# Mixture-of-experts stage of one fused kernel: the first two work items take their rows by gathers alone, with a spare gather ahead

## The reference

```python
# 1: attention, 4 batches x 8 heads x 576 rows, head_dim 64
scores = scale * q @ k.T
scores = where(scores >= max(scores) - tau, scores, -1e9)
x = softmax(scores) @ v                       # then reshaped to 2304 tokens x 512
# 2: mixture of experts, one expert of 8 for each token
logits = x @ w_gate                           # 512 x 8
expert_idx = argmax(logits, axis=1)
gate_w = softmax(logits)[expert_idx]
for e in range(8):
    xe = x[expert_idx == e]
    out[expert_idx == e] = gate_w * (relu(xe @ w1[e]) @ w2[e])   # 512x1024, 1024x512
# 3: dense layer
h = x @ w_in                                  # 512 x 2048
out = (h - tanh(h)) @ w_out                   # 2048 x 512
```

## Time and profile before

| what | value |
|---|---|
| runs of the kernel before, median (lowest to highest) | 1090.57 us (1089.77 to 1091.09) |
| the profiled execution, its own time | 1086.2 us |
| its span, from the first to the last instruction | 1084.1 us |
| mean granted PE clock in it, of full speed | 0.991 |
| PE busy | 1042.3 us, 96% of the span |
| DVE, ACT, POOL busy | 673.7, 469.0, 785.4 us |
| DMA traffic | 110.01 MB, mean 101 GB/s |

### The profile page before, as it was taken

How to read it: one execution, slowest core, us unless ns; L and a number is a source line. 1 busy time by engine, 2 the same in 40 slices (tenths; PEclk the granted TensorE clock), 3 DMA queues, 4 the chain that set the end, 5 groups by cost and what they waited for, 6 DMA issues and landing times.

```text
span 1084.1 us, 18472 instructions
## 1 busy us (share of the span) xinstructions
PE 1042.3 (96%) x5928; PEld 869.4 (80%) x5929; DVE 673.7 (62%) x1396; ACT 469.0 (43%) x945; POOL 785.4 (72%) x794
## 2 busy tenths in 40 slices
PE   6999999999995989999999999999999999999997
PEld 5767767777774778888888888999999999999995
DVE  5777777777786132322234226997777777777775
ACT  5777777777763122222222224433343333333332
POOL 4788888666632867967899803888878778787885
PEclk9999999999998999999999999999999999999999
DMA  6464575554532555635564521010000100000000
GB/s 120 112 173 127 149 207 119 159 133 110 152 113 68 201 193 178 209 126 194 179 214 171 210 79 58 1 31 10 20 30 27 33 10 21 30 20 11 11 20 29
DMA packets 100487, 110.01 MB, mean 101 GB/s; under 512 B 64896, under 2 KB 64896, under 8 KB 99904
## 3 DMA queue, kind: packets, MB, share of 16 engines
q1 hardware_dynamic: 88160, 85.73, 27.3%
q10 hardware_dynamic: 9136, 13.15, 3.8%
q0 software_dynamic: 3120, 10.24, 2.5%
HBM read 68.01 MB, written 27.32 MB: 88 GB/s over the span
## 4 chain that ended last, share of the span: by engine, by line
PE 78%; POOL 11%; issue 5%; DVE 3%; ACT 2%; DMA 1%; POOLq 0%; SPq 0%; ACTq 0%; DVEq 0%
PE ps L1150 19%; PE ps L1165 18%; PE ps L1131 12%; PE ps L1109 11%; PE ps L942 4%; PE ps L906 4%; PE ps L920 4%; POOL k_low L691 2%; PE ps L1119 2%; POOL q_dup L679 2%; POOL x_sorted L796 2%; POOL thresh L698 1%; POOL k_hl L689 1%; PE ps L928 1%; PE ps L969 1%
## 5 line engine op out<-in xcount | busy, mean ns | idle before, releaser
L835 POOL TENSOR_SCALAR x_sb<-h_sq 128x384 f32<-128x384 f32 x96 | 148.6, 1548 | 8.1
L1131 PE MATMUL ps<-ring,hT 128*128 x600 | 144.6, 397 | 3.6 <-POOL ring L652 3.4
L1109 PE MATMUL ps<-ring,xT 128*128 x600 | 142.6, 393 | 1.0 <-DVE xT L1441 0.8
L644 POOL TENSOR_TENSOR ring<-x_sb,ring 128x2048 fp32r<-128x2048 f32 x30 | 138.1, 4604 | 2.5
L1234 DVE SCALAR_TENSOR_TENSOR probs<-ps,thresh,probs 128x576 f32<-128x576 f32 x144 | 115.4, 811 | 38.5 <-ACT probs L1579 25.0
L1131 PEld LDWEIGHTS ps<-ring,hT 128*128 128x128 f32 x600 | 111.9, 190 | 26.8 <-issue 4.2
L832 POOL TENSOR_SCALAR poly<-h_sq 128x384 f32<-128x384 f32 x96 | 58.8, 613 | 99.5 <-ACT h_sq L1729 92.0
L1109 PEld LDWEIGHTS ps<-ring,xT 128*128 128x128 f32 x600 | 110.8, 188 | 23.2 <-issue 1.4
L906 PE MATMUL ps<-k_hl,q_dup 128*128 128x288 f32 (+1 forms) x640 | 117.3, 314 | 1.2 <-DVE probs L1234 1.1
L1226 DVE TENSOR_REDUCE neg_max<-ps 128x1 f32<-128x576 f32 x144 | 106.6, 749 | 13.4 <-PE ps L906 13.1
L834 POOL TENSOR_TENSOR poly<-poly,h_sq 128x384 f32<-128x384 f32 x96 | 104.6, 1089 | 8.0
(11 more groups left out here) (186 smaller groups left out, 1806.8 us busy)
## 6 DMA issues: line engine op xcount, KB each, us to landing
x_sb<-in_moe_w_dram SPq DMA_DIRECT2D x26, 1024.0 KB, 6.1
q_dup<-q_dup SPq DMA_DIRECT2D x30, 288.0 KB, 3.9
y_ranked<-y_sb ACTq DMA_DIRECT2D x25, 256.5 KB, 3.6
x_sorted<-y_sb SPq DMA_DIRECT2D x12, 514.0 KB, 5.3
xs<-x_sorted ACTq DMA_DIRECT2D x22, 257.0 KB, 2.8
k_hl<-k_low SPq DMA_DIRECT2D x30, 160.0 KB, 2.4
v_in<-in_v_dram SPq DMA_DIRECT2D x32, 128.0 KB, 2.6
raw_early<-in_moe_w_dram SPq DMA_DIRECT2D x16, 256.0 KB, 3.7
```

Of the source, the lines that this page charges most:

```text
L644: pool.tensor_tensor(ring[:, low:low + CHUNK], raw, ring[:, high:high + CHUNK].bitcast(F32), ALU.subtract).then_inc(w_ready, 1)
L835: pool.tensor_scalar(is_large[:, b, :], h_sq[:, b, :], T_SQ, None, ALU.is_ge).then_inc(large_ready, 1)
L1109: mm = pe.matmul(psS[:, 0, n, :], xT[:, px, c * P:(c + 1) * P], ring[:, bass.ds(lo + (pw * SLOT + c * F + n * 512), 512)], start=(c == 0 a ...
L1131: mm = pe.matmul(psO[:, 0, :], hT[:, px, c * P:(c + 1) * P], ring[:, bass.ds(lo + (pw * SLOT + DC * F + c * DM), DM)], start=(c == 0 and p ...
```

## The change

Four items instead of three are gathered from `x_tokens`; the fourth gather goes between the sixth and the seventh scatter, into part of `poly`. Before the gathers POOL issues a spare one of the first 128 token rows, with indices that DVE copied from the partition numbers, into the same part of `poly`, as soon as `x_tokens` is written and the first six `lanes` are made; the fourth gather waits for it. Item 0 has a row buffer of its own, `xT_first`, and a bank of its own for its result, `psO[:, 1]`. PE transposes item 1's rows between the two halves of `up(0)`, and ACT makes their high part between the two halves of `relu(0)`. On PE `down(0)` and `down(1)` no longer wait for `y_ready`. On ACT and DVE the work for items 1 and 2 (high_hT(1), relu(2), high_xT(3); low_hT(1), low_xT(3)) comes ahead of the wait for `x_scattered` and of `copy_y(0)`; `copy_y(0)` and `copy_y(1)`, and `store_rows(0)` and `store_rows(1)`, follow one another, and ACT's first load from `x_sorted` is that of item 4. The loops start at item 2. `meta` is loaded for four items.

```diff
@@ -53,7 +53,9 @@
     BPC = NB // CHUNKS
     PIECE = 512
     PIECES = CHUNK // PIECE
-    PICKED = 3
+    PICKED = 4
+    NEXT_PICKED = 3
+    SORTED_FIRST = 6
     LANE_GROUP = 6
     CLEARED = 2
     WARM_LOADS, WARM_SPLIT, WARM_ROWS, WARM_PICKED = 4, 4, 16, 8
@@ -216,7 +218,7 @@
-        xT, _, h_sb, hT = at_once([("xT", [P, 2, DM], F32R), ("x2T_rest", [P, 2 * DC * GW - 2 * DM], F32), ("h_sb", [P, F], F32), ("hT", [P, 2, F], F32R)])
+        xT, xT_first, _, h_sb, hT = at_once([("xT", [P, 2, DM], F32R), ("xT_first", [P, 2, DM], F32R), ("x2T_rest", [P, 2 * DC * GW - 4 * DM], F32), ("h_sb", [P, F], F32), ("hT", [P, 2, F], F32R)])

@@ -228,7 +230,9 @@
-        first_rows = [xs2[:, 0, 0:DM], xs2[:, 1, 0:DM], h_sq[:, :, :].rearrange("p b n -> p (b n)")[:, 0:DM]]
+        first_rows = [xs2[:, 0, 0:DM], xs2[:, 1, 0:DM]] + \
+            [x[:, :, :].rearrange("p b n -> p (b n)")[:, 0:DM] for x in (h_sq, poly)]
+        spare_rows = first_rows[NEXT_PICKED]

@@ -282,6 +286,8 @@
+        numbers_ready = sem("numbers_ready")
+        spare_landed = sem("spare_landed")

@@ -799,16 +805,27 @@
             pool.wait_ge(s_zero_filled, 16 * (-(-ITEMS // CLEARED)))
             pool.wait_ge(token_numbers, 5)
-            pool.wait_ge(x_kept, 32 * B)
-            pool.wait_ge(rows_ready, 1)
-            for t in range(PICKED):
+            def pick_rows(t):
                 pool.indirect_dma_start(
                     out=first_rows[t], out_offset=None, in_=x_tokens[:, :],
                     in_offset=bass.IndirectOffsetOnAxis(ap=item_rows[:, t:t + 1], axis=0)).then_inc(first_landed[t], 16)
+
+            pool.wait_ge(x_kept, 32 * B)
+            pool.wait_ge(numbers_ready, 1)
+            pool.wait_ge(lanes_ready, 1)
+            pool.indirect_dma_start(
+                out=spare_rows, out_offset=None, in_=x_tokens[:, :],
+                in_offset=bass.IndirectOffsetOnAxis(ap=token_u[:, 0:1], axis=0)).then_inc(spare_landed, 16)
+            pool.wait_ge(rows_ready, 1)
+            for t in range(NEXT_PICKED):
+                pick_rows(t)
             pool.wait_ge(x_ready, 2 * PAIRS)
             pool.wait_ge(pos_ready, 1)
             pool.wait_ge(gates_ready, 1)
             for t in range(TILES):
+                if t == SORTED_FIRST:
+                    pool.wait_ge(spare_landed, 16)
+                    pick_rows(NEXT_PICKED)
                 sort_tile(t)
             for j in range(CHUNKS, EARLY):
                 split_mid(j)
@@ -1101,12 +1118,15 @@
                     pe.wait_ge(xT_high, t + 1)
                 else:
                     pe.wait_ge(xT_ready, t + 1)
+                rows = xT_first if first else xT
                 for n in range(F // 512):
+                    if n == 1 and between is not None:
+                        turn_rows(between, first_rows[between])
                     for px, pw in PASSES:
                         if first and px == 1:
                             pe.wait_ge(xT_ready, t + 1)
                         for c in range(DC):
-                            mm = pe.matmul(psS[:, 0, n, :], xT[:, px, c * P:(c + 1) * P],
+                            mm = pe.matmul(psS[:, 0, n, :], rows[:, px, c * P:(c + 1) * P],
                                            ring[:, bass.ds(lo + (pw * SLOT + c * F + n * 512), 512)],
                                            start=(c == 0 and px + pw == 0), stop=(c == DC - 1 and px == 1))
                     mm.then_inc(h_psum, 1)
@@ -1119,16 +1139,16 @@
                         mm = pe.transpose(psS[:, 1, n, c * P:(c + 1) * P], h_sb[:, f:f + P], ident[:, :])
                     mm.then_inc(hT_psum, 1)
-            def down(t, first=False):
+            def down(t, to=0, clear=True):
                 e = pe.value_load(item_e_i[0:1, bass.ds(t, 1)], min_val=0, max_val=E - 1)
                 lo = pe.snap((e % 2) * (2 * SLOT))
                 pe.wait_ge(w_ready, (e + 1) * CHUNKS)
-                if not first:
+                if clear:
                     pe.wait_ge(y_ready, t)
                 pe.wait_ge(hT_ready, 2 * t + 2)
                 for c in range(FC):
                     for px, pw in PASSES:
-                        mm = pe.matmul(psO[:, 0, :], hT[:, px, c * P:(c + 1) * P],
+                        mm = pe.matmul(psO[:, to, :], hT[:, px, c * P:(c + 1) * P],
                                        ring[:, bass.ds(lo + (pw * SLOT + DC * F + c * DM), DM)],
                                        start=(c == 0 and px + pw == 0), stop=(c == FC - 1 and px == 1))
                 mm.then_inc(items_done, 1)
@@ -1182,13 +1202,16 @@
             pe.wait_ge(row0_ready, 1)
             turn_rows(0, first_rows[0])
             keep_warm(WARM_PICKED).then_inc(rows_warm, 1)
-            up(0, first=True)
-            turn_rows(1, first_rows[1])
+            up(0, first=True, between=1)
             turn_hidden(0)
             up(1)
             turn_rows(2, first_rows[2])
-            down(0, first=True)
-            with pe.Fori(1, ITEMS - 2) as t:
+            down(0, to=1, clear=False)
+            turn_hidden(1)
+            up(2)
+            turn_rows(3, first_rows[3])
+            down(1, clear=False)
+            with pe.Fori(2, ITEMS - 2) as t:
                 turn_hidden(t)
                 up(t + 1)
                 turn_rows(t + 2)
@@ -1339,6 +1362,8 @@
+                    dve.wait_ge(s_const, 14)
+                    dve.tensor_copy(token_u[:, 0:1], partition_no[:, :]).then_inc(numbers_ready, 1)

@@ -1443,11 +1468,12 @@
-            def low_xT(t, picked=False):
+            def low_xT(t, picked=False, first=False):
-                low_of(xT[:, 1, :], psT[:, 0, :], xT[:, 0, :]).then_inc(xT_ready, 1)
+                rows = xT_first if first else xT
+                low_of(rows[:, 1, :], psT[:, 0, :], rows[:, 0, :]).then_inc(xT_ready, 1)

@@ -1462,7 +1488,7 @@
-                dve.tensor_scalar(y_sb[:, 0:DM], psO[:, 0, :], of_item(t, 0), None, ALU.mult).then_inc(y_ready, 1)
+                dve.tensor_scalar(y_sb[:, 0:DM], psO[:, 1 if first else 0, :], of_item(t, 0), None, ALU.mult).then_inc(y_ready, 1)

@@ -1516,12 +1542,15 @@
                     if g + 1 < NG and b in TURN_AT:
                         low_x2T(g + 1, TURN_AT.index(b))
-            low_xT(0, picked=True)
+            low_xT(0, picked=True, first=True)
             low_xT(1, picked=True)
             low_hT(0)
             low_xT(2, picked=True)
+            low_hT(1)
+            low_xT(3, picked=True)
             copy_y(0, first=True)
-            with dve.Fori(1, ITEMS - 2) as t:
+            copy_y(1)
+            with dve.Fori(2, ITEMS - 2) as t:
                 low_hT(t)
                 low_xT(t + 2)
                 copy_y(t)
@@ -1687,12 +1716,14 @@
-            def high_xT(t):
+            def high_xT(t, first=False):
-                act.activation(xT[:, 0, :], psT[:, 0, :], ACT.Copy).then_inc(xT_high, 1)
-
-            def relu(t):
+                act.activation((xT_first if first else xT)[:, 0, :], psT[:, 0, :], ACT.Copy).then_inc(xT_high, 1)
+
+            def relu(t, between=None):
+                    if n == 1 and between is not None:
+                        high_xT(between)

@@ -1764,16 +1795,19 @@
             act.wait_ge(map_ready, 2)
             act.wait_ge(row0_ready, 1)
-            high_xT(0)
-            relu(0)
-            high_xT(1)
+            high_xT(0, first=True)
+            relu(0, between=1)
             high_hT(0)
             relu(1)
             high_xT(2)
+            high_hT(1)
+            relu(2)
+            high_xT(3)
             act.wait_ge(x_scattered, 16 * TILES)
-            load_rows(3)
+            load_rows(4)
             store_rows(0)
-            with act.Fori(1, ITEMS - 3) as t:
+            store_rows(1)
+            with act.Fori(2, ITEMS - 3) as t:
                 high_hT(t)
                 relu(t + 1)
                 high_xT(t + 2)
```

More of the change, by code:

```diff
@@ L1094, in turn_rows, with up @@
                 mm.then_inc(xs_trans, 1)
-            def up(t, first=False):
+            def up(t, first=False, between=None):
                 e = pe.value_load(item_e_i[0:1, bass.ds(t, 1)], min_val=0, max_val=E - 1)
```

## The result

The changed kernel took 1094.67 us (median of 12 runs, 1092.87 to 1096.67 but for one disturbed run of 2623.09), the kernel before 1090.38 us (12 runs, 1088.41 to 1093.20). The ratio is 1.0039, with a 95% interval of 1.0029 to 1.0049: slower by 4.3 us, where 4.6 us less was forecast.

The account below looks back on a forecast made before the run. PE was taken as the bound, busy for 1042.3 of 1084.1 us. Gather 0.9, order of item 1 0.6 and third and fourth loss 6.2, less 3.1 of new wait, gave 4.6 off the median: 1086.0 us, range 1082.6 to 1088.9.

Parts of the forecast that it names:

- up(1) starts 7.3 after up(0): PE, item 1: relu(0)'s second half ends 6.83 after up(0) starts, then four hidden transposes (0.44); before it was 7.91.
- the wait for the store: Ahead of down(2): copy_y(1) waits for store 0, since `y_sb` is one buffer; 3.1 us taken off the gains.
- Gather, 0.9 gained: POOL: the spare pays the first gather's long start, so gather 0 runs from 346.4 to 347.4, ending 0.9 earlier.
- Order of item 1, 0.6 gained: Item 1's rows transposed between the halves of up(0): up(1) starts 7.3 after up(0) instead of 7.91, 0.6 gained.
- Down(1) at 377.0 at full clock: PE: down(1) starts at 377.0 without its wait and ends at 382.5 instead of 390.24, 7.75 gained.
- The new wait: Store 0 lands at 388.0, copy_y(1) ends at 388.9, down(2) starts at 392.1; PE idle for some 2.7 us.
- Its clock: down(2) counted at full clock, 5.74 us, since the 2.7 us idle is less than 3.45, after which the clock fell.
- rival B: The clock falls in the hole before down(2), which pays 1.5: 3.1 gained, 1087.5 us; chance 0.17.
- Rival E: Each transfer on ACT's queue waits the full 7.2 us in turn; down(2) ends 2.2 later than before, 1092.8 us; chance 0.06.

Follow-up runs that it names:

- r1_before: The kernel before, unchanged, run again on the first chip for a second profile: 1090.20 us (0.9993 of its own runs beside it).
- r3_before: The kernel before, unchanged, run again on the second chip: 1085.90 us, and 1084.28 in its 25 runs beside.
- r1_no_spare: The changed kernel without the spare gather and the copy of its indices, first chip: 1091.66 us (1.0009 of before).
- r3_after: The changed kernel, unchanged, on the second chip: 1083.94 us (0.9992 of before).
- r3_padded: The changed kernel with 40 increments of an unused semaphore on ACT and 48 on PE ahead of the first item, second chip: 1086.19 us.
- r5_paced: The changed kernel with an own buffer for item 0's result and at most two scatters in flight, fourth chip: 1082.53 us (0.9925 of before).
- r4_own_result: The changed kernel with item 0's result in a buffer of its own, so copy_y(1) doesn't wait for store 0, third chip: 1093.46 us (1.0034 of before).
- r5_in_order: The changed kernel with indirect scatters to rows in token order, last stores writing whole tiles, sort left out, fourth chip: 1092.16 us (1.0012 of before).
- r4_dve_first: r4_own_result with ACT's work for items 0 to 3 ahead of the wait for the scatters done by DVE, third chip: 1094.69 us (1.0039 of before).
- r4_pool_copies: The changed kernel with the scatters as plain whole-tile copies issued by POOL, last stores writing whole tiles, sort left out, third chip: 1079.84 us.

## Why the prediction was wrong, point by point

**The step that failed** is one that the sum has at nothing: that ACT, DVE and PE take up their work promptly while 18 scatters run beside. On three of the four chips they don't, and no rival named it. In the sum's own terms it breaks first at "up(1) starts 7.3 after up(0)": in the result's profile up(1) starts 21.8 us after up(0) (351.97 to 373.76), since the second relu, forecast to end 6.83 after up(0), ends 20.6 after it (372.57). So down(1) starts at 393.38 instead of 377.0, and the wait for the store, the largest term that was taken off, is not on the path at all.

The sign of it was in the last sentence of the sum: "The profiled execution was 1086.2, 4.4 under the median of 1090.57; I take the difference off the median". The 4.4 us were in view and were passed over. They say that the runs lose something that the profiled execution doesn't, and nearly all of it can lie in the stretch that the change rebuilds: r1_before's profiled execution took 4.8 us more than r3_before's (1090.70 and 1085.87), and its turn_hidden(3) started 4.9 later. The profile from which I predicted looks like one of a chip like the second: its 1086.2 us and its down(1) at 382.98 stand beside 1085.87 and 382.58 in r3_before, while its kernel's three runs, from 1089.77 to 1091.09, look like those of the other chips. No chip is noted for either, so this is likely and not shown.

**Gather, 0.9 gained**: right in itself. On the second chip PE's first transposes came 0.77 earlier (349.82 against 350.59), in the result's profile at 349.52. The long start did belong to the first use: gather 0 takes 1.06 behind the spare and 1.23 without it (r1_no_spare). What the sum lacks is its price on the first chip, where the kernel without the spare is 2.7 us faster. The Trainium skill (GPSIMD Engine Reference, section Instruction dispatch) has the first call of a freshly loaded kernel cost about 6 us. The trace disagrees again, with the spare started at 344.03 and done by 345.26.

**Order of item 1, 0.6 gained**: wrong by 0.86. In r3_after up(1) starts 8.16 us after up(0), where 7.3 was forecast and r3_before has 7.86. After turn_hidden(0) PE waits 0.62 for nothing that is shown, and between its two halves PE now waits 0.25 for the second relu.

**Down(1) at 377.0 at full clock**: right in kind on the second chip, at 377.83 with 5.75; the 0.83 are the step before.

**The new wait**: right on the second chip. Copy_y(1) starts at 388.79 where the store was forecast to land at 388.0, and down(2) at 392.54 instead of 392.1.

**Its clock**: rival B came true on the second chip. I counted the hole at full clock because it was shorter than the 3.45 of the earlier trace rows. It was 2.19, and yet the granted clock over the first 3 us of down(2) was 0.66: the window from 392.60 to 395.60 of r3_after, with the columns of the earlier trace rows:

```profile
392.60:395.60 3.00, 3.00 (x9) 2.43 (x10) 2.58 (x1) 0.26 (x1) 3.00 (x1) 0.66 0.00 0
```

It is a mean of the two levels of 1.2 and 2.4 GHz: 0.99 until 393.60 and 0.50 from there to 396.60, so the clock fell one microsecond after PE had gone back to work. Down(2) took 1.6 us more than down(1) just before. A hole of 1.18 in r3_padded left it at 5.75, one of 0.37 in r5_paced at 5.74.

**In sum, on the second chip**: 2.2 us less by the profiled executions (1081.6 against 1083.8), 4.6 less 1.6 for the clock and 0.86 for the order. By the medians it is 0.3 against the 25 runs beside and 2.0 against the ten of r3_before: the runs of before there fall into two groups, near 1084.0 and near 1085.9, and the profiled one belongs to the upper. Over all 35 the mean is 1085.1, 1.0 above the mean of after (1084.1), so the change gains about 1 us there. What parts the groups no profile shows; a lower clock doesn't, for the mean granted clock was 0.990 in each run of the faster group and 0.991 on average in the slower.

**Rival E**, the slower one, had the right sign for a wrong reason: with the holes, the copy and store of item 0 are off the path. In the result's profile copy_y(1) ends at 399.91 and hT(2) is split by 402.54, 3.1 us before down(2) takes it.

What stays open is the mechanism between the scatters and the engines. Shown is, on chips where before takes some 1090: beside unpaced indirect scatters ACT (r4_own_result, r5_in_order), DVE (r4_dve_first) and PE (r1_before) are held up; beside plain copies of the same bytes at a higher rate they are not (r4_pool_copies), and beside scatters with two in flight they are not (r5_paced). And the chips differ, though the scatters run alike: 211 GB/s at a DMA share of 0.56 from 351 to 373 us in r1_before, 210 and 0.56 in r3_before. The profile has no row for what the engines lack. The fetches of instructions that it does show (one of 8 KB, one of 16 KB) lie at 350 to 353 and at 354 to 357 us in the kernels before and after on both kinds of chip, and none lies between 357 and 377 in a profile with holes, so they don't explain it. The Trainium skill (DMA: Bandwidth & Descriptors, section Back-pressure in remote DMA) says of transfers from one core to another that stalled writes stall the other queues of the source DMA engine too, and that the fetching of descriptors stalls once writes stop flushing. The transfers here stay on one core, and no run shows whether anything like it happens.

## What to carry to other kernels

Ask of a profiled execution that lies outside its kernel's runs where the difference is, before taking a sum against it: a stretch that waits in most runs has hidden slack in one kernel and none in the next, and a change that removes slack pays for every hold-up. Beside latency-bound work on other engines, try indirect scatters of many rows with two in flight, if what waits for them has room; here the kernel that had this and the own buffer was 8 us faster than before on one chip. And where an experiment is to tell two theories apart, run the kernel before beside it on the same chip and look whether it shows the effect at all; two of these series did not.

## What was not expected of the hardware

- Chips differ in how prompt engines are beside scatters: the same kernel before took 1084.3 us on one of four chips and 1089.8 to 1090.8 on the three others, while a kernel without scatters beside the items took the same on two of them, one of either kind (1079.82 and 1079.84).
- Eighteen indirect scatters at a DMA share of 0.57 held engines up for up to 13.4 us, where plain copies of the same bytes, in the same number of packets, at a share of 1.05 did not.
- PE can stand still inside a series of matmuls that wait for nothing (three holes of 1.02 to 1.67 us inside down(0) of r1_before).
- PE's granted clock fell after an idle stretch of 2.19 us, one microsecond into the matmuls that followed, which took 1.6 us more; after 1.18 us idle they took no more.
- Slowing the scatters down (one every 1.73 us instead of 1.28) took the kernel with the own buffer from 1.0034 of before on one such chip to 0.9925 on another, some 12 us, while the change itself moved 4.
